# Attention scores as three products over 64 rows, the halves of the keys side by side in the array, in place of four products over 128 rows

## What is computed

```
scores = q @ k.T / sqrt(64)                        # 576 x 576 per head, 32 heads
keep   = scores >= max(scores, axis=-1) - tau
attn   = exp(scores - max) * keep;  attn /= sum(attn) + 1e-9
x      = attn @ v                                  # heads side by side: 2304 x 512
h      = x @ w_in;    x = relu(h)**2 @ w_out               # 512 -> 2048 -> 512
h      = x @ w2_in;   out = (h * tanh(softplus(h))) @ w2_out
```

## Time and profile before

| | before |
|---|---|
| median of 3 runs | 1183.61 us (1182.19 to 1185.51) |
| profiled execution | 1182.92 us, of which span 1181.1 us |
| PE busy | 1114.6 us, 94% of the span |
| PE weight loads busy | 1047.8 us |
| DVE, ACT, POOL busy | 776.3, 641.5, 569.3 us |
| mean granted clock of PE | 0.987 |

### The profile page before, as it was taken

The page is one execution under the profiler, slowest core; times in us unless marked ns, Lnnn a source line. Parts: engine busy times, 40 slices in busy tenths (PEclk is TensorE's granted clock), DMA queues, the critical chain, the costliest instruction groups (busy, mean ns, idle before and its releaser), DMA issues.

```text
span 1181.1 us, 21018 instructions
## 1 busy us (share of the span) xinstructions
PE 1114.6 (94%) x7472; PEld 1047.8 (89%) x7472; DVE 776.3 (66%) x2009; ACT 641.5 (54%) x1214; POOL 569.3 (48%) x641
## 2 busy tenths in 40 slices
PE   5776789999999999999999999989999999999998
PEld 4565589999999999999999999978999999999997
DVE  4666677767766777677660102478877787878776
ACT  4555556565656665656553334555555555555554
POOL 3555467767676767776654444512222222222222
PEclk9989889999999999999999999989999999999999
DMA  4333232212221212122101302520100101010000
GB/s 136 102 107 108 78 97 66 69 52 72 56 61 50 76 43 69 52 73 58 40 18 39 99 1 73 169 72 1 54 1 1 54 1 54 1 54 1 28 1 27
DMA packets 73545, 65.33 MB, mean 55 GB/s; under 512 B 26081, under 2 KB 58849, under 8 KB 73441
## 3 DMA queue, kind: packets, MB, share of 16 engines
q1 hardware_dynamic: 68528, 58.98, 17.5%
q10 hardware_dynamic: 4912, 5.01, 1.3%
HBM read 49.81 MB, written 14.16 MB: 54 GB/s over the span
## 4 chain that ended last, share of the span: by engine, by line
PE 83%; DVE 6%; ACT 4%; issue 3%; DMA 2%; SPq 0%; POOL 0%; POOLq 0%; ACTq 0%; DVEq 0%
PE acc L130 8%; PE acc L131 8%; PE acc L132 8%; PE hidden L130 6%; PE hidden L132 6%; PE hidden L131 6%; PE pT L932 6%; PE scores L921 3%; PE pT L130 3%; PE pT L132 3%; PE pT L131 3%; PE scores L922 3%; PE outs L961 3%; PE outs L962 3%; PE scores L130 3%
## 5 line engine op out<-in xcount | busy, mean ns | idle before, releaser
L528 POOL TENSOR_TENSOR g_lo<-g,g_hi 128x384 fp32r<-128x384 f32 x96 | 97.7, 1018 | 314.1 <-ACT g_hi L559 314.1
L505 POOL TENSOR_SCALAR probs<-probs,inv_sum,flat 128x576 f32<-128x576 f32 x144 | 120.4, 836 | 184.3 <-DVE inv_sum L769 183.8
L130 PE MATMUL hidden<-x_hi,w_hi 128*128 128x256 f32 x576 | 170.9, 297 | 2.2 <-DVE x_lo L803 1.6
L130 PE MATMUL acc<-g_hi,w_hi 128*128 128x256 f32 x576 | 164.1, 285 | 0.0
L131 PE MATMUL acc<-g_lo,w_hi 128*128 128x256 f32 x576 | 163.1, 283 | 0.0
L132 PE MATMUL acc<-g_hi,w_lo 128*128 128x256 f32 x576 | 163.0, 283 | 0.0
L132 PE MATMUL hidden<-x_hi,w_lo 128*128 128x256 f32 x576 | 162.9, 283 | 0.0
L131 PE MATMUL hidden<-x_lo,w_hi 128*128 128x256 f32 x576 | 162.7, 282 | 0.0
L733 DVE TENSOR_SCALAR_CACHE_REDUCE s_neg<-scores 128x576 f32<-128x576 f32 x126 | 94.9, 753 | 74.0 <-PE scores L922 73.8
L518 POOL TENSOR_TENSOR rg<-rg 128x256 f32<-128x256 f32 x144 | 99.8, 693 | 75.7 <-ACT rg L626 74.7
L593 ACT ACTIVATE probs<-s_neg,neg_top 128x576 f32<-128x576 f32 x144 | 110.4, 767 | 13.9 <-DVE s_neg L733 13.7
(11 more groups left out here) (116 smaller groups left out, 3119.0 us busy)
## 6 DMA issues: line engine op xcount, KB each, us to landing
k_raw<-kT SPq DMA_DIRECT2D x64, 144.0 KB, 2.9
q_raw<-qT SPq DMA_DIRECT2D x62, 144.0 KB, 3.0
y<-w_in SPq DMA_DIRECT2D x26, 256.0 KB, 2.8
y<-w_out SPq DMA_DIRECT2D x26, 256.0 KB, 3.4
x_raw<-x SPq DMA_DIRECT2D x36, 128.0 KB, 2.1
x<-y ACTq DMA_DIRECT2D x9, 512.0 KB, 2.9
x_raw<-x SPq DMA_DIRECT2D x6, 768.0 KB, 5.2
out<-y SPq DMA_DIRECT2D x18, 256.0 KB, 2.3
```

The costliest lines, as they stand in the source:

```text
L130: pe.matmul(out, a_hi, b_hi, start=first, stop=False, **flags)
L505: pool.tensor_scalar(probs[:, t, :], probs[:, t, :], inv_sum[:, t:t + 1], flat[:, t:t + 1], ALU.mult, ALU.add).then_inc(probs_ready, 1)
L528: pool.tensor_tensor(g2_lo[:, k % GRING, :], g2[:, k % 2, :], g2_hi[:, k % GRING, :].bitcast(F32), ALU.subtract).then_inc(g2_split, 1)
```

## The change

The split no longer takes the second half of the partitions. The queries' parts are two tiles, `q_hi` and `q_lo`, each with the same 64 rows on both halves of the partitions. The keys' parts are halved: keys 0 to 287 stand on partitions 0 to 63 and keys 288 to 575 on 64 to 127, so `k_raw`, `k_hi` and `k_lo` have 288 columns instead of 576. A product over partitions 0 to 63 makes the scores of the first half of the keys into one PSUM bank, one over 64 to 127 those of the second half into the other. Three parts are summed, q_hi k_hi + q_hi k_lo + q_lo k_hi; the product of the two low parts is left out. With two halves that is six products of 64 rows and 288 columns per block, alternating between the halves of the array.

POOL's `split_queries` now works on all 128 partitions, writes to its own tile, and no longer waits for `probs_ready` ahead or `q_ready` behind. Two more memsets clear the zero columns of `q_lo`. The keys' transfers are of half the size, in the same number and order.

```diff
--- before.py
+++ after.py
@@ -166,13 +166,16 @@
         pt_hi = early("pt_hi", [P, QT, 3 * P], F32R)
         pt_lo = early("pt_lo", [P, QT, 3 * P], F32R)
         q_raw = early("q_raw", [P, SEQ])
-        k_raw = early("k_raw", [P, SEQ])
+
+        k_raw = early("k_raw", [P, HALF])
 
         v_raw = early("v_raw", [P, 2, QT + 1, HD])
 
-        q_split = early("q_split", [P, 2, SEQ + HD], F32R)
-        k_hi = early("k_hi", [P, 2, SEQ], F32R)
-        k_lo = early("k_lo", [P, 2, SEQ], F32R)
+
+        q_hi = early("q_hi", [P, 2, SEQ + HD], F32R)
+        q_lo = early("q_lo", [P, 2, SEQ + HD], F32R)
+        k_hi = early("k_hi", [P, 2, HALF], F32R)
+        k_lo = early("k_lo", [P, 2, HALF], F32R)
         v_split = early("v_split", [P, 2, QT, 2 * HD], F32R)
         s_neg = early("s_neg", [P, 2, SEQ])
         probs = early("probs", [P, PRING, SEQ])
@@ -349,7 +352,8 @@
                     sp.wait_ge(q_ready, h)
                 for half in range(2):
                     rows = slice(half * HD, (half + 1) * HD)
-                    sp.dma_start(k_raw[rows, :], kT[h * HD:(h + 1) * HD, :]).then_inc(k_loaded, 16)
+                    sp.dma_start(k_raw[rows, :], kT[h * HD:(h + 1) * HD, half * HALF:(half + 1) * HALF]
+                                 ).then_inc(k_loaded, 16)
                     if h > 0:
                         sp.dma_start(q_raw[rows, :], qT[h * HD:(h + 1) * HD, :]).then_inc(q_loaded, 16)
 
@@ -474,8 +478,9 @@
         def _(pool):
             pool.memset(v_raw[0:HD, :, QT - 1, :], 0.0).then_inc(v_clear, 1)
             pool.memset(v_raw[:, :, QT, :], 0.0).then_inc(v_clear, 1)
-            pool.memset(q_split[:, 0, SEQ:SEQ + HD].bitcast(F32), 0.0).then_inc(q_clear, 1)
-            pool.memset(q_split[:, 1, 0:HD].bitcast(F32), 0.0).then_inc(q_clear, 1)
+            for q in (q_hi, q_lo):
+                pool.memset(q[:, 0, SEQ:SEQ + HD].bitcast(F32), 0.0).then_inc(q_clear, 1)
+                pool.memset(q[:, 1, 0:HD].bitcast(F32), 0.0).then_inc(q_clear, 1)
             pool.memset(ident[:, :], 0.0).then_inc(ident_ready, 1)
             pool.wait_ge(ident_ready, 1)
             pool.affine_select(out=ident[:, :], in_=ident[:, :], compare_op=ALU.not_equal, fill=1.0,
@@ -486,13 +491,10 @@
                 pool.tensor_tensor(k_lo[:, h % 2, :], k_raw[:, :], k_hi[:, h % 2, :].bitcast(F32),
                                    ALU.subtract).then_inc(k_ready, 1)
 
-            def split_queries(h, s):
-
-                pool.wait_ge(probs_ready, s)
+            def split_queries(h):
                 pool.wait_ge(q_high, h + 1)
-                q = q_split[HD:P, h % 2, query_columns(h)]
-                pool.tensor_tensor(q, q_raw[HD:P, :], q.bitcast(F32), ALU.subtract).then_inc(q_ready, 1)
-                pool.wait_ge(q_ready, h + 1)
+                pool.tensor_tensor(q_lo[:, h % 2, query_columns(h)], q_raw[:, :],
+                                   q_hi[:, h % 2, query_columns(h)].bitcast(F32), ALU.subtract).then_inc(q_ready, 1)
 
             def split_values(h):
                 pool.wait_ge(v_high, h + 1 - HEADS)
@@ -534,7 +536,7 @@
                 if s in KEYS_AT:
                     split_keys(KEYS_AT[s])
                 if s in QUERIES_AT:
-                    split_queries(QUERIES_AT[s], s)
+                    split_queries(QUERIES_AT[s])
                 if s in VALUES_AT:
                     split_values(VALUES_AT[s])
                 if s in WEIGHTS_AT:
@@ -566,7 +568,7 @@
 
             def high_queries(h):
                 act.wait_ge(q_loaded, 32 * (h + 1))
-                copy(q_split[:, h % 2, query_columns(h)], q_raw[:, :]).then_inc(q_high, 1)
+                copy(q_hi[:, h % 2, query_columns(h)], q_raw[:, :]).then_inc(q_high, 1)
 
             def high_values(h):
                 act.wait_ge(v_loaded[h % 2], 32 * (h // 2 + 1))
@@ -683,7 +685,7 @@
             for half in range(2):
                 act.dma_start(q_raw[half * HD:(half + 1) * HD, :], qT[0:HD, :]).then_inc(q_loaded, 16)
             high_keys(0)
-            act.wait_ge(q_clear, 2)
+            act.wait_ge(q_clear, 4)
             high_queries(0)
             for s in range(SLOTS):
                 c = chunk_weighed(s - 1)
@@ -854,8 +856,8 @@
             dve.tensor_tensor(k_lo[:, 0, :], k_raw[:, :], k_hi[:, 0, :].bitcast(F32), ALU.subtract
                               ).then_inc(k_ready, 1)
             dve.wait_ge(q_high, 1)
-            dve.tensor_tensor(q_split[HD:P, 0, query_columns(0)], q_raw[HD:P, :],
-                              q_split[HD:P, 0, query_columns(0)].bitcast(F32), ALU.subtract).then_inc(q_ready, 1)
+            dve.tensor_tensor(q_lo[:, 0, query_columns(0)], q_raw[:, :],
+                              q_hi[:, 0, query_columns(0)].bitcast(F32), ALU.subtract).then_inc(q_ready, 1)
             dve.wait_ge(tau_loaded, 16)
             for s in range(SLOTS):
                 if s < TILES:
@@ -894,7 +896,7 @@
         @block.tensor
         def _(pe):
             pe.wait_ge(ident_ready, 2)
-            pe.wait_ge(q_clear, 2)
+            pe.wait_ge(q_clear, 4)
 
             def score_tile(n):
                 p, j = n // PER, n % PER
@@ -913,13 +915,13 @@
                 parts = [(0, P * j)] if j <= MIXED else [(1, P * (j - MIXED))]
                 if j == MIXED:
                     parts = parts + [(1, 0)]
-                for half in range(2):
-                    keys = slice(half * HALF, (half + 1) * HALF)
-                    out = scores_of(n)[:, half, 0:HALF]
-                    for u, at in parts:
-                        q = q_split[:, u, at:at + P]
-                        pe.matmul(out, q, k_hi[:, u, keys], start=(u, at) == parts[0], stop=False)
-                        mm = pe.matmul(out, q, k_lo[:, u, keys], start=False, stop=(u, at) == parts[-1])
+
+                products = [(q, k, u, at) for u, at in parts for q, k in ((q_hi, k_hi), (q_hi, k_lo), (q_lo, k_hi))]
+                for i, (q, k, u, at) in enumerate(products):
+                    for half in range(2):
+                        rows = slice(half * HD, (half + 1) * HD)
+                        mm = pe.matmul(scores_of(n)[:, half, 0:HALF], q[rows, u, at:at + P], k[rows, u, :],
+                                       start=i == 0, stop=i == len(products) - 1)
                 mm.then_inc(scores_ready, 1)
 
             def transposes(n):
```

## The result

| | before | after |
|---|---|---|
| median of 4 runs | 1184.56 us (1182.19 to 1186.69) | 1203.20 us (1201.11 to 1203.57) |
| profiled execution | 1182.92 us, span 1181.1 | 1203.09 us, span 1201.3 |

The ratio is 1.0154, with a 95% interval of 1.013 to 1.0178: slower by 18.6 us. The forecast was 1204.0 us. The number is right, and the mechanism that it was worked out from is not: the products of a pair run side by side, their weight loads too, and what is lost is lost at the changes between 128 and 64 rows.

A forecast was written before the change was run, and what follows sets the result against it. PE's instructions were taken to bound the late stretch and the chain through the score products the early one; 14.6 late + 7.5 early - 1 preparation = +21.1 us on 1182.9 gave 1204.0 us, range 1196 to 1212 (8 in 10: 1160 to 1227).

The forecast's parts named there:

- What bounds the kernel: Late, time is the sum of PE's instructions; early, the chain through the score products moves it nearly one to one.
- the first rival: In the score block, both halves' products and weight loads run fully side by side: -23 us, 1160 us; chance 0.33.
- the chain's 17.9%: Early stretch: score products' waits hold 17.9%, or 28 us, of the chain, so block length moves time nearly one to one.
- What comes: Score block of three pairs over 64 rows: products overlap, loads follow each other, 0.66 us a block, +0.13 us; chance 0.34.
- 0.177 us: Time of a pair of products in the score block below which the forecast is wrong; 0.53 / 3.
- The term of +14.6 us late: Late stretch: 112 blocks, each 0.13 us longer because a pair's weight loads follow each other.
- the second rival: Array empties at each change between 128 and 64 rows, twice a tile: 1199 us, or 1221 if loads wait; chance 0.18.
- Break-even: Changes between 128 and 64 rows around the score block cost more than all of the gain from 73 ns each upwards.
- Preparation: Copying and splitting keys and queries ahead of the scores gets cheaper with half-width keys: -1 us, within 0 and -3.
- The sum: Whole kernel: 14.6 late + 7.5 early - 1 for cheaper key and query splitting = +21.1 us, giving 1204.0 us.
- A range with both signs: Whole kernel's range for 8 in 10: 1160 to 1227 us, holding both faster and slower outcomes.
- the chance of 0.34: Chance given to the forecast's own case in the score block: products of the halves overlap, weight loads one after another.

The follow-up runs named there:

- with six products: The kernel after, but each of its six products per block reads all 128 rows instead of 64: 1214.9 us, ratio 1.0281.
- with three products: The kernel after, but each block made of only three products over all 128 rows: 1171.0 us, ratio 0.9897.
- four products: The kernel after, its preparation and layout kept, but each block made of four products over all 128 rows: 1183.8 us, ratio 1.0001.
- a single and a pair: The kernel before with one extra product over 64 rows, or a pair on both halves, ahead of each score tile: 1239.0 and 1237.3 us.
- two and four blocks in a row: Both kernels with each block's products issued 2 or 4 times: before 1249.25 and 1405.20 us, after 1254.32 and 1364.48 us.
- grouped order: The kernel after with the three products of rows 0 to 63 first, then the three of rows 64 to 127: 1208.6 us, ratio 1.0223.

## Why the prediction was right in its number and wrong in its mechanism

*What bounds the kernel.* Right for the late stretch where the block gets longer: there the change went into the time at nearly its full size (26.9 of 114 x 0.265 = 30.2 us with six products), and 20.2 of the 20.2 us of span lie there. For a shorter block it is wrong, "a nanosecond taken from" PE was not "a nanosecond of the kernel": with three products the late stretch gave back 7.9 of 15.1 us. So the first rival's 1160 us was probably out of reach even with free changes; the kernel with three took 1171 (no run removed the changes of rows from pairs; three products over all rows stand for them). The early stretch was read wrongly. The forecast took the chain's 17.9% as "nearly one to one". From four products to six over 128 rows with the same preparation, the early part grew by 5.2 us (-0.4 to +4.8), where 46 blocks of 0.30 us would have made 13.8; from four to three it fell by 4.2 us of 46 x 0.15 = 6.9. The medians say the same (1214.9 - 1183.8 = 31.1 us, of which 25.6 late). PE's waits for the mask get shorter as its work gets longer: 39.6 us with four and 34.7 with six. The profiled execution with six also had a higher clock early than before had (0.92):

```profile
7.00:163.00 156.00, 117.97 (x627) 98.13 (x628) 95.74 (x350) 75.80 (x117) 75.26 (x71) 0.96 0.32 92
```

But other executions of that kernel had the mean clock of before (0.987) over the whole span, and this one 0.993, so how much of the early difference is the clock's is not shown.

*What comes.* This is the step that failed: "the products of the halves overlap, but their loads do not". The reading of the load behind it was sound (0.11 us and 0.21 us), and it is seen again in after: 303.20 to 303.31, over 64 rows the same as over 128. The step from there, that two loads for different halves follow each other, had no row behind it, and the pairs of loads refute it. A pair takes 0.13 us, less than the 0.177 us that the prediction itself named as the sign of being wrong. The term of +14.6 us late does not exist. In its place stand -15.1 us for the pairs and +35.3 us for the changes, of which the second rival named both parts, the tail (0.16 us each) and the open load (0.11 us). With both it gave 1221 us: 0.27 us a change, when two cost 0.343 together. The measured time lies between its 1199 us (the tail alone) and its 1221 us (both). The forecast of that rival took the whole shown tail of a product; the load going in starts when 0.09 of it is over (0.21 - 0.12).

*Break-even.* The rival's point, 73 ns a change, was passed: a change costs 0.17 us, so the changes outweigh the gain. Here the rule of the Trainium skill (TensorEngine Tiling (Array Packing), Key Properties: a change of tiling mode drains the engine) was the one that decided, and the trace agrees, with 0.21 us from a product's start to the next load where a change lies between. The other rule of the same section of the Trainium skill, that tiles load and multiply in parallel, agrees as well: a single and a pair cost the same.

*Preparation.* Forecast -1 us (0 to -3). By itself it measured nothing (ratio 1.0001), early -0.4 us. Its parts came as worked out: the keys' copy fell to 432 ns (430 forecast), their rest on POOL to 804 (820), and the queries' rest stayed with twice the partitions:

```profile
L496 POOL TENSOR_TENSOR q_lo<-q_raw,q_hi 128x576 fp32r<-128x576 f32 x31 | 45.4, 1463 | 3.2 <-ACT q_hi L561 3.0
...
L491 POOL TENSOR_TENSOR k_lo<-k_raw,k_hi 128x288 fp32r<-128x288 f32 x31 | 24.9, 804 | 9.6 <-ACT k_hi L561 9.6
...
L561 ACT ACTIVATE k_hi<-k_raw 128x288 fp32r<-128x288 f32 x32 | 13.8, 432 | 3.6 <-DMA k_raw<-kT 3.6
```

The first product starts 0.5 us sooner than in the earlier trace rows, at 6.86 us:

```profile
6.86 0.61 PE L923 MATMUL scores<-k_hi,q_hi 64*128 64x288 f32 x2 [6.86 <-DVE q_lo L859]
```

*The sum.* +14.6 late, +7.5 early, -1 became +20.2, +1.9 and -0.4, with -1.5 us behind attention, which is noise. That the sum came within 1 us was luck: the errors cancelled, a late term too small by 5.6 us and an early one too large by as much, and an early difference of 1 or 2 us is itself hardly clear of noise. A range with both signs was honest, but the chance of 0.34 stood on the wrong case; the true one had 0.18.

## What to carry to other kernels

Two products over 64 rows on different halves of the array cost as one, loads included, but going from 128 rows to 64 and back cost 0.34 us of the kernel's time here (0.35 to 0.40 of PE's), as much as 2.6 products of 288 columns. Count the changes before the products: packing loses when each short block stands alone between full products. Here the sign turned between two and four blocks in a row, at 35.3 / 15.1 = 2.3 by the late figures (worked out, not run at 3). A share of a chain in a stretch where the engine also waits is not a slope; a kernel with one more product in it measures the slope.

## What the runs showed of the hardware

- Two products over different halves of the array run at the same time, with their loads: the second one of a pair added nothing (1239.0 and 1237.3 us).
- The tail and load at a change: the load behind it starts 0.21 us after the start of the last product of 256 columns, and its own 0.11 us are no longer hidden.
- PE takes products of the idle half of the array ahead of waiting ones of the other: grouped order cost 0.40 us only where six stood in a row. The order of products in the program is not the order of their starts.
- The way in cost the same 0.09 us (0.21 in place of 0.12) and the load wherever it was looked at; the way out cost 0.15 us ahead of transposes and 0.20 ahead of products with the values (320 columns). What stays open: how the cost depends on the width of the products beside the change; no run varied it.
